# Eight 64x32 tiles in place of two 128x64 tiles for the values times w_in, in the attention's PSUM banks

## The reference

```python
a   = softmax(phi)                                  # b h s m, m = 32
k_m = einsum('bhsm,bhsd->bhmd', a, k)
v_m = einsum('bhsm,bhsd->bhmd', a, v)
p   = softmax(q @ k_m.T / 8)                        # b h s m
x   = (p @ v_m) -> [b*s, h*d]
h   = x @ w1_in ;  g = where(h > 0, h, exp(min(h, 0)) - 1) ;  x = g @ w1_out
h   = x @ w2_in ;  g = h * clip(h + 3, 0, 6) / 6          ;  out = g @ w2_out
```

## Time and profile before

| | |
|---|---|
| median of 3 runs | 1638.16 us (1637.02 to 1641.31) |
| the profiled execution's own time | 1637.58 us |
| span of its trace | 1635.8 us |
| granted TensorE clock, mean | 0.997 of full speed |
| TensorE busy | 1579.6 us, 97% |
| VectorE busy | 659.4 us, 40% |
| ScalarE busy | 654.2 us, 40% |
| GpSimd busy | 132.2 us, 8% |
| units 0 to 15 (layer 1) | from about 45 us to about 838 us |

### The profile page before, as it was taken

How to read it: one execution, slowest core, us unless ns; L and a number is a source line. 1 busy time by engine, 2 the same in 40 slices (tenths; PEclk the granted TensorE clock), 3 DMA queues, 4 the chain that set the end, 5 groups by cost and what they waited for, 6 DMA issues and landing times.

```text
span 1635.8 us, 25445 instructions
## 1 busy us (share of the span) xinstructions
PE 1579.6 (97%) x9840; PEld 1364.1 (83%) x9840; DVE 659.4 (40%) x1163; ACT 654.2 (40%) x1363; POOL 132.2 (8%) x99
## 2 busy tenths in 40 slices
PE   4999999999999999999999999999999999999999
PEld 3788989879888798888998888888888888888887
DVE  4455555554555545555353232232323232323222
ACT  2565555545555455555573222222222222222222
POOL 0320000000000000000182101010101010101000
PEclk9899999999999999999999999999999999999999
DMA  9423221232212222120321010101010101010000
GB/s 246 136 42 66 52 59 42 47 68 52 59 38 52 64 55 59 38 52 17 143 79 65 0 52 0 52 0 51 0 51 0 51 0 51 0 49 2 7 19 26
DMA packets 178101, 79.50 MB, mean 49 GB/s; under 512 B 152400, under 2 KB 160592, under 8 KB 178000
## 3 DMA queue, kind: packets, MB, share of 16 engines
q1 hardware_dynamic: 168528, 76.07, 17.6%
q10 hardware_dynamic: 9472, 2.07, 0.8%
HBM read 59.24 MB, written 18.87 MB: 48 GB/s over the span
## 4 chain that ended last, share of the span: by engine, by line
PE 57%; issue 37%; DVE 2%; ACT 2%; POOL 1%; ACTq 1%; POOLq 0%; DVEq 0%
PE ps L281 18%; PE ps L283 18%; PE ps L282 18%; POOL rows L724 1%; PE ps L352 1%; DVE g L640 1%; PE ps L331 1%; ACT g_hi L503 0%; PE ps L302 0%; ACT g L501 0%; ACT g L499 0%; DVE g_lo L642 0%; ACTq L556 0%; PE ps L320 0%; ACTq L554 0%
## 5 line engine op out<-in xcount | busy, mean ns | idle before, releaser
L281 PE MATMUL ps<-g_hi,w_out_lo 128*128 128x288 f32 x1024 | 314.1, 307 | 0.9 <-POOL w_out_lo L713 0.6
L282 PE MATMUL ps<-g_lo,w_out_hi 128*128 128x288 f32 x1024 | 301.7, 295 | 0.0
L283 PE MATMUL ps<-g_hi,w_out_hi 128*128 128x288 f32 x1024 | 301.7, 295 | 0.0
L509 ACT ACTIVATE g<-ps,one_half 128x512 f32<-128x512 f32 x144 | 99.3, 690 | 465.6 <-PE ps L283 465.6
L648 DVE SCALAR_TENSOR_TENSOR g<-g,ps 128x512 f32<-128x512 f32 x144 | 99.2, 689 | 450.5 <-ACT g L509 450.5
L281 PE MATMUL ps<-x_hi,w_in_lo 128*128 128x512 f32 x576 | 224.1, 389 | 0.0
L283 PE MATMUL ps<-x_hi,w_in_hi 128*128 128x512 f32 x576 | 224.1, 389 | 0.0
L282 PE MATMUL ps<-x_lo,w_in_hi 128*128 128x512 f32 x576 | 224.1, 389 | 0.0
L281 PE MATMUL ps<-w_out_hi,g_lo 128*128 128x512 f32 x576 | 224.1, 389 | 0.0
L282 PE MATMUL ps<-w_out_lo,g_hi 128*128 128x512 f32 x576 | 224.1, 389 | 0.0
L283 PE MATMUL ps<-w_out_hi,g_hi 128*128 128x512 f32 x576 | 224.1, 389 | 0.0
(11 more groups left out here) (108 smaller groups left out, 1950.7 us busy)
## 6 DMA issues: line engine op xcount, KB each, us to landing
layer_out<-y_sb SPq DMA_DIRECT2D x16, 576.0 KB, 3.1
x_raw<-layer_out SPq DMA_DIRECT2D x9, 1024.0 KB, 6.9
kv<-in_k SPq DMA_DIRECT2D x60, 144.0 KB, 3.4
kv<-in_v SPq DMA_DIRECT2D x60, 144.0 KB, 3.5
q<-in_q SPq DMA_DIRECT2D x60, 144.0 KB, 2.9
w_in_raw<-in_moe_w_in SPq DMA_DIRECT2D x8, 1024.0 KB, 10.9
w_out_raw<-in_moe_w_out SPq DMA_DIRECT2D x8, 1024.0 KB, 6.2
out<-out_sb SPq DMA_DIRECT2D x8, 1024.0 KB, 5.1
```

Source lines behind the costliest of these rows:

```text
L281: nc.tensor.matmul(dst, a_lo, b_hi, start=first, stop=False)
L282: nc.tensor.matmul(dst, a_hi, b_lo, start=False, stop=False)
L283: return nc.tensor.matmul(dst, a_hi, b_hi, start=False, stop=last)
L509: nc.scalar.activation(g2[f % 2][:], hid(f, BLOCK), ACT.Relu, bias=one_half[:, 0:1], scale=1.0 / 6.0).then_inc(e_made, 1)
```

## The change: what it does

Groups are formed otherwise: group 0 of a batch holds the even heads and group 1 the odd ones, so that the 128 rows of one chunk of `w_in` belong to one head of each group. `vT` is a single 128x128 tile: partitions 0 to 63 are group 0's values, 64 to 127 group 1's, with no zeros. An item is now both groups at once: eight f32 matmuls with 64 contraction rows and 32 stationary columns each (64x32 tiles), 512 columns wide, into two banks. There are 4 items in a batch, 32 in all. They are written to the attention's banks 6 and 7 (the two in the ramp to banks 4 and 5), and no longer take turns in the `hid` banks. ScalarE makes two copies for each item and VectorE two subtractions, of the same shape as before, so that their number is the same.

The items stand at `f` = 9, 12, 15 of the odd units and at `f` = 1 of the next one (in unit 0 at 1 and 4). The stages of the attention move by a step from MAX on: 0, 2, 3, 5, 6, 7, 8, 10, 11, 12, 14. Since items and stages share banks, each waits for the other's readers: the waits in `item_banks` stand between the two halves of the `up1` ahead of an item, and a stage MAX, KV, SCORES or PT that comes one or two steps behind an item waits for `w1_lo_made`. SyncE loads the heads in the new order, with as many transfers of the same size.

```diff
-    PRE = 4
+    PRE = 2
-        STEP_OF = (0, 1, 2, 4, 5, 6, 7, 9, 10, 11, 13)
+        STEP_OF = (0, 2, 3, 5, 6, 7, 8, 10, 11, 12, 14)
         def items_in(u, parity):
             if isinstance(u, int) and u == 0:
-                return {0: 4, 1: 5, 2: 6, 3: 7}
+                return {1: 2, 4: 3}
...
-            return {6: 0, 7: 1, 9: 2, 10: 3, 12: 4, 13: 5} if parity else {0: 6, 1: 7}
+            return {9: 0, 12: 1, 15: 2} if parity else {1: 3}
-            def item(i, n, g, at, turn):
-
-                gi = n % 2
-                cols = slice(n // 2 * BANK, (n // 2 + 1) * BANK)
...
-                for p in range(2):
-                    lm = slice(p * 2 * M, (p + 1) * 2 * M)
-                    mm = nc.tensor.matmul(hid(at, BANK)[lm], vT[:, gi, lm], w_in_raw[:, 2 * gi + p, cols], start=True, stop=True)
+            def item(n, bank):
+
+                cols = slice(n * BANK, (n + 1) * BANK)
+
+                for h in range(MAC):
+                    for gi in range(2):
+                        rows, lm = slice(gi * DH, (gi + 1) * DH), slice(h * M, (h + 1) * M)
+                        mm = nc.tensor.matmul(ps[lm, bank + gi, 0:BANK], vT[rows, lm], w_in_raw[rows, h, cols],
+                                              start=True, stop=True)
                 mm.then_inc(item_done, 1)
+            def item_banks(u, f):
+
+                g = u + AHEAD
+                if f == 4:
+                    pe.wait_ge(a_sub_made, g + 1)
+                elif f == 9:
+                    pe.wait_ge(q_copied_act, nth(g, 1))
+                    pe.wait_ge(q_copied_dve, nth(g, 1))
+                elif f == 12:
+                    pe.wait_ge(p_sub_step, 2 * (g + 1))
+                elif f == 15:
+                    pe.wait_ge(pT_lo_made, g + 1)
+                elif f == 1 and beyond(u):
+                    pe.wait_ge(w1_lo_made, 2 * u + 3)
                 for gi in range(2):
-                    if f == 0 and parity == 0 and gi == 0:
-                        pe.wait_ge(pT_lo_made, u + 2)
+                    if gi == 1 and f in items:
+
+                        item_inputs(item_index(u, parity, items[f]), items[f], u + 2 + parity)
+                        item_banks(u, f)
                     if attend:
                         for stage in stages_at(f):
-                            attention(u + AHEAD, stage, A)
+                            behind = None
+                            for e in (f - 1, f - 2):
+                                if e in items and stage in (S_MAX, S_KV, S_SCORES, S_PT):
+                                    behind = item_index(u, parity, items[e]) + 1
+                            attention(u + AHEAD, stage, A, behind)
-            def item(i, n, at):
+            def item(i, n, bank):
                 act.wait_ge(item_done, i + 1)
-                nc.scalar.copy(w1_hi[n // 2][:, n % 2], hid(at, BANK)).then_inc(w1_hi_made, 1)
+                for gi in range(2):
+                    nc.scalar.copy(w1_hi[n][:, gi], ps[:, bank + gi, 0:BANK]).then_inc(w1_hi_made, 1)
+            def item(i, n, bank):
+                for gi in range(2):
+                    dve.wait_ge(w1_hi_made, 2 * i + gi + 1)
+                    op = nc.vector.tensor_tensor(w1_lo[n][:, gi], ps[:, bank + gi, 0:BANK], w1_hi[n][:, gi].bitcast(F32),
+                                                 ALU.subtract)
+                op.then_inc(w1_lo_made, 1)
```

More of the change, by code:

```diff
@@ L283, in three_passes, with attention @@
                 return nc.tensor.matmul(dst, a_hi, b_hi, start=False, stop=last)
-            def attention(g, stage, t):
+            def attention(g, stage, t, items=None):
+                if items is not None:
+                    pe.wait_ge(w1_lo_made, items)
                 if stage == S_MAX:
@@ L357, in up1 @@
+            def up1(u, f, parity, slots, items):
+                if beyond(u * FC + f - 1):
+                    pe.wait_ge(turn_over, u * FC + f - 1)
+                if f == 0 and parity == 0:
+                    pe.wait_ge(pT_lo_made, u + 2)
+                if f == 0 and not beyond(u):
+                    pe.wait_ge(w1_lo_made, PRE)
+                if f % FS == 0 and parity == 0:
+                    pe.wait_ge(w1_lo_made, 2 * u + f // FS + 1)
                 for gi in range(2):
-                    if f == 0 and parity == 0 and gi == 0:
-                        pe.wait_ge(pT_lo_made, u + 2)
+                    if gi == 1 and f in items:
+                        item_inputs(item_index(u, parity, items[f]), items[f], u + 2 + parity)
+                        item_banks(u, f)
@@ L404, in half @@
                 parity, first = um % 2, isinstance(u, int) and u == 0
[L405 to L408, removed]
+                items = items_in(u, parity)
+                for f in range(FC):
+                    up1(u, f, parity, um - parity, items)
+                    if f in items:
+                        item(items[f], ATT)
                     if attend:
                         for stage in stages_at(f):
-                            attention(u + AHEAD, stage, A)
+                            behind = None
[3 more added lines that the diff above has]
+                            attention(u + AHEAD, stage, A, behind)
                     if f >= LAG:
@@ L466, in attention @@
                     nc.scalar.mul(t.kmT, t.ps_kmT, SCALE).then_inc(kmT_copied, 1)
-                    nc.scalar.copy(vT[:, slot % 2], t.ps_vT).then_inc(vT_made, 1)
+                    rows = slice(gi * DH, (gi + 1) * DH)
+                    nc.scalar.copy(vT[rows], t.ps_vT[rows]).then_inc(vT_made, 1)
                 elif stage in (S_Q0, S_Q1):
@@ L523, in half @@
                 last = isinstance(u, int) and u == UNITS1 - 1
-                for f, at, n in turns(u, parity):
-                    step1(u, f, at, first_turn(u, parity) + at)
+                items = items_in(u, parity)
+                for f in range(FC):
+                    step1(u, f)
                     if f == LAG - 1 and not first:
                         leave(u - 1, y_sb)
-                    if n is not None:
-                        item(item_index(u, parity, n), n, at + 1)
+                    if f in items:
+                        item(item_index(u, parity, items[f]), items[f], ATT)
                     if attend:
@@ L562, in _ @@
                 if stage in (S_Q1, S_EXP):
-                    for n in ((0, 1) if stage == S_Q1 else (2, 3)):
-                        item(n, n, n)
+                    item(int(stage == S_EXP), int(stage == S_EXP), HID)
             half(0, 0, True)
@@ L664, in half @@
                 parity, first = um % 2, isinstance(u, int) and u == 0
-                for f, at, n in turns(u, parity):
-                    step1(u, f, at)
+                items = items_in(u, parity)
+                for f in range(FC):
+                    step1(u, f)
                     if f == LAG - 1 and not first:
                         leave(u - 1, y_sb)
-                    if n is not None:
-                        item(item_index(u, parity, n), n, at + 1)
+                    if f in items:
+                        item(item_index(u, parity, items[f]), items[f], ATT)
                     if attend:
@@ L691, in _ @@
                 if stage in (S_Q1, S_NORM):
-                    for n in ((0, 1) if stage == S_Q1 else (2, 3)):
-                        item(n, n, n)
+                    item(int(stage == S_NORM), int(stage == S_NORM), HID)
             half(0, 0, True)
@@ L741, in half @@
                 last = isinstance(u, int) and u == UNITS1 - 1
-                for f, _, n in turns(u, parity):
+                for f in range(FC):
                     if attend:
@@ L765, in _ @@
             for t in (A, B_):
-                nc.gpsimd.memset(t.kvm[:, 0:2], 0.0).then_inc(zeros_ready, 1)
+                nc.gpsimd.memset(t.kvm[:, 0:4], 0.0).then_inc(zeros_ready, 1)
             normalise(0, A)
```

136 lines of the change are left out of this document (62 added, 74 removed).

## The result

The changed kernel takes 1627.03 us in the median of 4 runs (1624.7 to 1630.34), the kernel before 1637.68 us: a ratio of 0.9934 with the interval [0.9919, 0.9948]. It is 10.6 us faster. The forecast was 28 us faster, with 1601 to 1629 as its range; the time lies in the range and the direction is right, but the gain is little more than a third of the one forecast.

A forecast was written before the change was run, and what follows sets the result against it. TensorE, busy 97%, was taken as the bound. Per set 4.2 (items) + 2.7 (waits gone) - 3.3 (waits new) = 3.6 us; seven sets 25.2, unit 14 0.6, ramp and unit 0 1.9: 28 us less, 1610 us, range 1601 to 1629.

The forecast's parts named there:

- Items: Small TensorE matmuls per set: eight items at 9.3 us become four at 1.27 us each, 5.1 us; 4.2 us less a set.
- Waits that go: TensorE's waits for PHI's maxima (odd unit), ahead of the item at 13, and for L587 (even unit) vanish: 2.7 us a set.
- Waits that come: New TensorE waits behind items, at SCORES, MAX, SUB, `up1` at 9 and PT: together 3.3 us a set.
- MAX in the even units: MAX at step 2, behind the item at 1, waits for VectorE's second subtraction: 1.4 us.
- the middle of `up1` at 9: TensorE waits between the halves of this `up1` for the copies of Q1 at 8: 0.35 to 0.4, taken as 0.4 us.
- PT in the odd units: PT at 14 waits for GpSimd's product as in the even unit, since the item at 12 cancels out: 0.8 us.
- Ramp: At the head of SCORES, two items taking 1.94 us become one of some 1.0: 0.9 us less.
- Unit 0: Four interruptions become two, saving 2 to 3 us; bank wait costs 1.2 and MAX about 1; taken as 1.0 us less.
- Layer 2 unchanged: Sign listed for the trace after the change: layer 2 stays as it was, with no term in the sum.
- Row groups in turns: TensorE's row groups alternate, so an item costs 2.13 us; gain 10 in all, 1628 us; chance 0.12.
- Rival 2: Copies out of the shared banks bound: four places cost 1 us more each, time 1638 us; chance 0.06, including half of it.

## Why the prediction missed

**Items.** Right. Row tiles run side by side as column tiles do; an item is 1.22 us where 1.27 was taken, four are 4.9, and a set gains 4.2 to 4.4 us by them (4.2 forecast). This was the open point of the forecast, and it fell at its cheap end.

**Waits that go.** Right: L290 on L583 is no longer among the larger waits of the main units, and the one ahead of the item at 13 went.

**Waits that come.** Right in place, small by a quarter in size: 3.3 us were worked out, 4.1 came. MAX in the even units 1.6 (1.4 forecast), the middle of `up1` at 9 0.44 (0.4), SCORES 0.37 (0.3), PT in the odd units 0.9 (0.8), MAX and SUB in the odd units 0.4 together (0.4, which was put on SUB alone; SUB's excess is 0.36 us there and was 0.39 before). KMT in the even units waits 0.4 us for ScalarE's copy of `kvm`, which I had not looked at. A set came to 3.1 us less and not 3.6. That is some 3 us of the shortfall over all sets.

**Ramp.** 0.9 us were forecast and 0.2 came in these two traces. Among the traces of all versions the first `up1` starts anywhere from 43.5 to 46.7 us, so that neither number says much.

**Unit 0.** Wrong in sign: +4.7 in place of -1.0. I put MAX behind the item at about 1 us; TensorE was idle for 2.9 us there, since VectorE stood first at PHI, which ended at 50.7 us, before it came to that item's `w_lo`:

```profile
53.40 0.42 PE L275 MATMUL ps<-ident,kvm 96*128 96x96 f32 x1 [2.87 <-DVE w_lo L657]
```

And NORM came a step later, with GpSimd's product 5.3 us later than before (92.87 and 87.60 us); the remaining splits of `w_out`, one for each step, queue behind it on GpSimd. But the larger part is the clock, for which the sum had no term. The kernel before takes 54.8 us here. The changed order takes 55.9 us in the two traces without half clock between 52 and 100 us (the one with TensorE's loops written out, and that with groups outer, whose code differs only in the order within an item), 57.5 us with one stretch of 3.4 us, and 59.5 with 6.8 and 3.4. So of the 4.7 us some 3.6 go with the clock and 1.1 with the order. Why the stretches come in one execution and not in another stays open.

**Code.** This is the step that failed most: the sum had no term for it. "Layer 2 unchanged", and a sum without a line for the loops, took the pauses at the jumps for a constant. Between the traces they are 8.5 us dearer after the change: 5.2 in layer 1, of which 3.4 by the clock behind them, and 3.3 in layer 2. The rows of the kernel before told of them: a pause of 1.76 us at 354 us, in which TensorE waited for nothing that the profile could name, under `issue`. The prediction gives it no word.

**Rivals.** Row groups in turns would have given 1628 us, which is within 1 us of what was measured, by another cause. The item of 1.22 us rules it out. A time that fits a rival is not evidence for it. Rival 2 is out by the waits, which came to 4.1 us a set. That the time lies within the range is luck: the range was made for dearer items and longer waits, and losses that the sum did not have used it up.

Of 27.7 us forecast 21.4 are there with the loops of three engines written out, and 10.6 with the jumps. What is left without jumps is 3 us in the sets' waits and, by the traces, 3.5 in unit 0 (2.5 lost in place of 1.0 gained, of which 1.6 by the one stretch at half clock).

## What to carry to other kernels

Here tiles of 64x32 in two row groups and four column groups cost what two tiles of 128x64 did: fill the array with small products wherever both dimensions allow it, and sum the break (0.35 us) once for a pack. Results that share banks with other stages buy this with waits; put the wait for the bank as late as it can stand, directly ahead of the writer. And before an edit in a kernel with hardware loops is judged by its time, look for pauses at the jumps and for the clock behind them, or compare both versions with the loops written out: here the same edit is worth 10.6 us or 21.4. Look at the clock ahead of the loops as well: all but the same code took 59.5 us around unit 0 in one execution and 55.9 in another.

## What the runs showed of the hardware that was not expected

- A shift of TensorE's code by 128 instructions made the changed kernel 7.2 us faster (1619.78 against 1627.03 us) though it added work, and did not make the kernel before faster (1640.57 us).
- In the changed kernel idling of 2.38 and 2.44 us was followed by 3.4 us at 1.2 GHz. Idling of 1.47 to 1.59 us at the same places was not, in the kernel before and in the changed one with its code moved. With TensorE's loops written out one pause of 2.69 us was followed by it and one of 2.47 us was not: the length alone does not tell.
- Each engine pays for its own jump: with TensorE's loop gone ScalarE idled for 3.2 us at 355 us in the kernel before, and VectorE for 2.4 us at 347 us in the changed one.
- Sixteen f32 records of 512 columns on eight tiles lie within 1.09 us, and a second pack of eight adds 0.86 us.
